# Top-32 attention and two gated blocks on one core: direct and parked tiles alternate, a second tile's down products raw, w_out split later, three places for parked scores, other orders at the start and at the end of the first block

## The reference, cut to what is computed

```python
# q, k, v: [2, 8, 576, 64]
scores = (1 / 8) * q @ k.T                      # per head, 576 x 576
kth = 32nd largest of each row
scores = where(scores >= kth, scores, -1e9)
attn = softmax(scores) ; attn_out = attn @ v
x = attn_out as [1152 tokens, 512]
h = x @ w_in                                    # 512 x 2048
y = (max(h, 0) + alpha * min(h, 0)) @ w_out     # 2048 x 512
out = ((y @ w_a) * (y @ w_b)) @ moe2_w_out      # 512 x 1536 twice, 1536 x 512
```

## Time and profile before

| | us |
|---|---|
| median of 3 runs | 652.87 |
| profiled execution | 652.81 |
| its span | 651.0 |
| DVE busy | 425.1 (65%) |
| PE busy | 606.1 (93%) |
| ACT busy | 355.6 (55%) |
| POOL busy | 291.6 (45%) |

### The profile page before, as it was taken

One profiled execution on the slowest core, in us unless ns is written; L12 is line 12 of the kernel. 1 busy time (PEld: TensorE's weight loads), 2 busy tenths in 40 slices (PEclk: granted clock), 3 DMA queues, 4 the chain that ended last, 5 costly groups with the idle time before them and its releaser, 6 DMA issues.

```text
span 651.0 us, 10894 instructions
## 1 busy us (share of the span) xinstructions
PE 606.1 (93%) x4192; PEld 507.2 (78%) x4192; DVE 425.1 (65%) x847; ACT 355.6 (55%) x642; POOL 291.6 (45%) x285
## 2 busy tenths in 40 slices
PE   5588789998999999999898989999999999999997
PEld 4366566676777878777776867899999999999996
DVE  4999999999899999999999006554221122212111
ACT  3498987877777776776676645553222112121111
POOL 0266689899978898878868660000000000000000
PEclk9877999999999999999999999999999999999999
DMA  8899972223113424332340352730011000010001
GB/s 266 316 308 350 328 267 63 73 72 87 42 59 92 132 81 127 114 112 76 114 123 29 113 167 81 263 125 1 1 49 49 0 1 1 0 50 1 0 1 48
DMA packets 30914, 68.06 MB, mean 105 GB/s; under 512 B 2704, under 2 KB 7312, under 8 KB 30736
## 3 DMA queue, kind: packets, MB, share of 16 engines
q1 hardware_dynamic: 30864, 67.38, 31.5%
HBM read 53.22 MB, written 14.16 MB: 103 GB/s over the span
## 4 chain that ended last, share of the span: by engine, by line
PE 50%; DVE 36%; POOL 8%; issue 3%; ACT 2%; DMA 1%; SPq 0%; ACTq 0%; POOLq 0%
DVE top L699 19%; DVE work L707 17%; PE ps L961 8%; PE ps L959 8%; PE ps L960 8%; PE ps L973 4%; PE ps L974 4%; PE ps L972 4%; POOL p_sb L431 2%; POOL wout_lo L418 2%; PE ps L859 2%; PE ps L861 2%; PE ps L860 2%; PE ps L891 2%; PE ps L894 1%
## 5 line engine op out<-in xcount | busy, mean ns | idle before, releaser
L699 DVE MAX8 top<-work 128x8 f32<-128x576 f32 x216 | 152.1, 746 | 0.0
L431 POOL TENSOR_TENSOR p_sb<-s_sb,p_sb 128x576 f32<-128x576 f32 x72 | 101.9, 1428 | 20.9 <-ACT p_sb L533 20.9
L752 DVE TENSOR_TENSOR ab<-ps,a_sb 128x384 f32<-128x384 f32 x36 | 20.1, 558 | 134.3 <-PE ps L961 134.3
L707 DVE MATCH_REPLACE8 work<-top,work 128x576 f32<-128x576 f32 x144 | 105.9, 744 | 0.0
L959 PE MATMUL ps<-y_parts,wab 128*128 128x384 f32 x288 | 97.2, 338 | 0.0
L961 PE MATMUL ps<-y_parts,wab 128*128 128x384 f32 x288 | 96.6, 336 | 0.0
L960 PE MATMUL ps<-y_parts,wab 128*128 128x384 f32 x288 | 96.4, 335 | 0.0
L539 ACT ACTIVATE p_sb<-p_sb,neg_max 128x576 f32<-128x576 f32 x72 | 56.3, 782 | 50.6 <-POOL p_sb L431 50.6
L859 PE MATMUL ps<-win_hi,xT_parts 128*128 128x512 f32 x144 | 59.6, 414 | 9.4 <-POOL xT_parts L448 7.3
L533 ACT ACTIVATE p_sb<-s_sb,kth_big 128x576 f32<-128x576 f32 x72 | 55.4, 787 | 11.3 <-POOL neg_max L426 11.3
L668 ACT ACTIVATE ab_hi<-ab 128x384 fp32r<-128x384 f32 x36 | 18.9, 525 | 78.0 <-DVE ab L752 78.0
(11 more groups left out here) (88 smaller groups left out, 1352.3 us busy)
## 6 DMA issues: line engine op xcount, KB each, us to landing
v_sb<-in_v SPq DMA_DIRECT2D x36, 320.0 KB, 2.9
s_dram<-keep_sb SPq DMA_DIRECT2D x16, 576.0 KB, 4.5
s_sb<-s_dram SPq DMA_DIRECT2D x16, 576.0 KB, 3.7
k_sb<-in_kT SPq DMA_DIRECT2D x24, 288.0 KB, 3.8
win_raw<-in_w_in SPq DMA_DIRECT2D x4, 1024.0 KB, 7.3
wout_raw<-in_w_out SPq DMA_DIRECT2D x4, 1024.0 KB, 9.0
wab_raw<-in_w_a SPq DMA_DIRECT2D x8, 384.0 KB, 4.0
wab_raw<-in_w_b SPq DMA_DIRECT2D x8, 384.0 KB, 6.0
```

Of the source, the lines that this page charges most:

```text
L431: nc.gpsimd.tensor_tensor(p_sb[:, chain.par, c, :], s_sb[:, chain.slot, c, :], p_sb[:, chain.par, c, :], ALU.subtract).then_inc(masked, 1)
L699: largest = nc.vector.max(top32[:, pair.par, c, 8 * r:8 * r + 8], work[:, c, :] if r else s_sb[:, pair.slot, c, :])
L707: nc.vector.match_replace(work[:, c, :], top32[:, pair.par, c, 8 * r:8 * r + 8], work[:, c, :] if r else s_sb[:, pair.slot, c, :], -3.0e38)\
```

## The change

1. **Order of the tiles.** `KINDS = "DSDPDPDPP"`: direct whole tile, split tile, then direct and parked ones in turn. Direct pairs are now 0 to 11, 16 to 19 and 24 to 27; parked ones 12 to 15, 20 to 23 and 28 to 35.
2. **Three places** for parked scores (`SLOTS = 3`). The third reaches into alpha's place, so alpha is loaded in SP's step 5 instead of 4, behind out2, once all parked stores have landed. ACT's `evict_x_turn(0)` waits for them too. `q_sb` moves behind `x_sb`.
3. **Raw down products** for the first two tiles (`RAW = 8`).
4. **w_out split** in ACT's steps 11 to 16 (POOL's 12 to 17) instead of 7 to 12 (8 to 13).
5. **Start.** Pair 0 is whole: its q is loaded first, then the two halves of its K (one per head) as two loads; its two heads go to places in different banks; the products of head 0 come first, with a semaphore of their own, and ACT copies head 0 from there.
6. **End of the first block.** `turn_x(8)` goes ahead of `down(30)`. For the last four quarters DVE computes slope and sum straight from PSUM, two operations instead of ACT's two and its own two; `halves_of_h` is gone there. The turns of y and `turn_g(35)` go ahead of the last two down products, and the last quarter's parts of g are written to the place of xT.

```diff
+RAW = 8
...
-DIRECT = (1 + WHOLE) * PAIRS
-KEPT = N_PAIRS - DIRECT
-SLOTS = 2
+KINDS = "DSDPDPDPP"
+DIRECT_PAIRS = [PAIRS * t + p for t in range(TILES) if KINDS[t] != "P" for p in range(PAIRS)]
+PARKED = [PAIRS * t + p for t in range(TILES) if KINDS[t] == "P" for p in range(PAIRS)]
+KEPT = len(PARKED)
+SLOTS = 3
...
-W_OUT_AT = {7: [0], 8: [1], 9: [2, 3], 10: [4], 11: [5, 6], 12: [7]}
-LOADS_AT = {-1: ["in1"], 0: ["in2"], 1: ["in3"], 2: ["out0"], 3: ["out1"], 4: ["alpha", "out2"], 5: ["out3"]}
+W_OUT_AT = {11: [0], 12: [1, 2], 13: [3], 14: [4, 5], 15: [6], 16: [7]}
+LOADS_AT = {-1: ["in1"], 0: ["in2"], 1: ["in3"], 2: ["out0"], 3: ["out1"], 4: ["out2"], 5: ["alpha","out3"]}
+SPLIT = KINDS.index("S")
...
-                self.split = self.tile == 0
+                self.split = self.tile == SPLIT
...
-                self.kept = number - DIRECT if number >= DIRECT else None
+                self.kept = PARKED.index(number) if number in PARKED else None
+                self.nth = DIRECT_PAIRS.index(number) if number in DIRECT_PAIRS else None
...
+        def parts_for(seq):
+
+            return (xT_hi, xT_lo) if seq == LAST_SEQ else (g_hi, g_lo)
...
                 if what == "alpha":
+                    for slot in range(SLOTS):
+                        sp.wait_ge(kept_saved[slot], 16 * len(range(slot, KEPT, SLOTS)))
                     sp.dma_start(alpha_sb[:, :], alpha).then_inc(alpha_in, 16)
...
-            for p in range(KV):
-                load_kq(pair(p))
-                load_k1(p)
-            load_qa(WHOLE + 1)
-            for p in range(KV, PAIRS):
+            sp.dma_start(q_sb[:, 0, :], qT[0]).then_inc(q0_in, 16)
+            sp.dma_start(k_sb[0:D, 0, :], kT[0, 0, 0:D]).then_inc(k0_half_in, 16)
+            sp.dma_start(k_sb[D:P, 0, :], kT[0, 0, D:P]).then_inc(kq_in[0], 16)
+            load_kq(pair(1))
+            load_k1(0)
+            load_qa(0)
+            for p in range(1, PAIRS):
                 load_k1(p)
...
-                pool.wait_ge(down_done, c // 2 + 1)
+                pool.wait_ge(down_done, RAW - QUADS + c // 2 + 1)
...
-                if turning(i) is not None and turning(i) >= QUADS:
+                if turning(i) is not None and turning(i) >= RAW:
                     lo_of_g(turning(i))
...
+                elif tile == 0:
+                    for slot in range(SLOTS):
+                        act.wait_ge(kept_saved[slot], 16 * len(range(slot, KEPT, SLOTS)))
                 nc.scalar.activation(xT_hi, src, ACT.Copy)
...
-                halves_of_h(seq)
                 if seq == LAST_UP + 1:
                     evict_y(TILES - 2)
                 hi_of_w2(2 * (seq - LAST_UP - 1) + 1)
+                if seq == LAST_SEQ:
+                    for k in range(DC):
+                        hi_of_y(0, k, FIRST_Y[k])
                 parts_of_g(seq)
-            for k, bank in enumerate((U, 1, 2, 3)):
-                hi_of_y(0, k, bank)
...
-                dve.wait_ge(u_free, up_use(seq) + 1)
-                nc.vector.tensor_tensor(neg[:, :], neg[:, :], alpha_sb[:, q * 512:(q + 1) * 512], ALU.mult)\
-                  .then_inc(slope_done, 1)
+                dve.wait_ge(u_full, up_use(seq) + 1)
+                dve.wait_ge(gt_full, seq)
+                dve.wait_ge(sum_done, LAST_UP + 1)
+                nc.vector.scalar_tensor_tensor(neg[:, :], ps[:, U, :], 0.0, alpha_sb[:, q * 512:(q + 1) * 512],
+                                               ALU.min, ALU.mult).then_inc(slope_done, 1)
                 dve.wait_ge(slope_done, seq + 1)
-                nc.vector.tensor_tensor(pos[:, :], pos[:, :], neg[:, :], ALU.subtract).then_inc(sum_done, 1)
+                nc.vector.scalar_tensor_tensor(pos[:, :], ps[:, U, :], 0.0, neg[:, :],
+                                               ALU.max, ALU.add).then_inc(u_free, 1)
...
+                if pair.number == 0:
+                    parts = ((0, 0, CUT), (0, CUT, S), (1, S - CUT, S), (1, 0, S - CUT))
+                    pe.wait_ge(k0_half_in, 16)
+                    pe.wait_ge(q0_in, 16)
...
-            down(LAST_UP - 1)
-            turn_x(TILES - 1)
-            turn_g(LAST_UP)
-            for seq in range(LAST_UP + 1, LAST_SEQ + 1):
-                up(seq)
-                down(seq - 1)
-                turn_g(seq)
...
+            turn_x(TILES - 1)
+            down(LAST_UP - 1)
+            turn_g(LAST_UP)
+            for seq in range(LAST_UP + 1, LAST_SEQ):
+                up(seq)
+                down(seq - 1)
+                turn_g(seq)
+            up(LAST_SEQ)
+            for k in range(DC):
+                turn_y(0, k, FIRST_Y[k])
+            turn_g(LAST_SEQ)
+            down(LAST_SEQ - 1)
             down(LAST_SEQ)
```

More of the change, by code:

```diff
@@ L200, in __init__ @@
                 self.tile, self.hp = divmod(number, PAIRS)
-                self.split = self.tile == 0
+                self.split = self.tile == SPLIT
                 self.j = (self.tile + 1) % 2
-                self.batch = 0 if self.split else (self.tile - 1) // WHOLE
+                self.batch = 1 if KINDS[self.tile] == "P" else 0
                 self.par, self.bound = number % 2, number % 4
-                self.slot, self.kv, self.use = number % RING, number % KV, number // KV + 1
-                self.kept = number - DIRECT if number >= DIRECT else None
+                self.slot, self.v, self.use = number % RING, number % KV, number // KV + 1
+                self.kept = PARKED.index(number) if number in PARKED else None
+                self.nth = DIRECT_PAIRS.index(number) if number in DIRECT_PAIRS else None
+                self.kv = self.nth % KV if self.kept is None else None
+                self.loads = len([m for m in PARKED if m <= number and m % RING == self.slot])
         def pair(number):
@@ L211, in direct @@
         def direct(i):
-            return Pair(i + 3) if i + 3 < DIRECT else None
+            return Pair(i + 3) if i + 3 in DIRECT_PAIRS else None
         def score_order():
@@ L218, in score_order @@
             for i in range(FIRST_STEP, LAST_STEP):
-                order += [(i + 3, 0)] if i + 3 < DIRECT else []
-                order += [(DIRECT + n, 1 - at % 2) for at, n in enumerate(AHEAD.get(i, []))]
+                order += [(i + 3, 0)] if i + 3 in DIRECT_PAIRS else []
+                order += [(PARKED[n], 1 - at % 2) for at, n in enumerate(AHEAD.get(i, []))]
             before = {}
@@ L255, in up_use, with tiles_of @@
             return (1 + QUADS) * (seq // QUADS) + 1 + seq % QUADS
+        def parts_for(seq):
+            return (xT_hi, xT_lo) if seq == LAST_SEQ else (g_hi, g_lo)
         def row(tile):
-            return (tile - 1) * P if tile else SPLIT_AT
+            if tile == SPLIT:
+                return SPLIT_AT
+            return (KINDS[:tile].count(KINDS[tile]) + (WHOLE if KINDS[tile] == "P" else 0)) * P
+        def tiles_of(t):
+            return [tile for tile in range(TILES) if row(tile) // N2 == t]
         LAST_SEQ = TILES * QUADS - 1
+        FIRST_Y = (1, 2, 3, U)
         def w2_chunk(c):
@@ L351, in _ @@
                     load_v(pair(i + 1))
-                if i > FIRST_STEP and i + 5 < DIRECT:
-                    sp.wait_ge(scored, i + 4)
+                if i > FIRST_STEP and i + 5 in DIRECT_PAIRS:
+                    sp.wait_ge(scored, pair(i + 5).nth - 1)
                     load_kq(pair(i + 5))
@@ L376, in _ @@
             sp.wait_ge(u_full, turn_use(TILES - 1) + 1)
-            for tile in range(1, 1 + TILES2):
+            for tile in tiles_of(0):
                 sp.wait_ge(y_saved[tile], 16)
@@ L389, in _ @@
                 sp.wait_ge(y_turned, t * DC)
-                for tile in ((4, 5, 6), (7, 8, 0))[t - 1]:
+                for tile in tiles_of(t):
                     sp.wait_ge(y_saved[tile], 16)
@@ L508, in copy_scores @@
                 at = SC[0]
[L509 removed]
+                act.wait_ge(scored, pair.nth + 1)
                 if pair.number >= RING:
@@ L572, in halves_of_h @@
                     for slot in range(SLOTS):
-                        act.wait_ge(kept_saved[slot], 16 * KEPT // SLOTS)
+                        act.wait_ge(kept_saved[slot], 16 * len(range(slot, KEPT, SLOTS)))
                 nc.scalar.activation(pos[:, :], ps[:, U, :], ACT.Relu)
@@ L691, in rank @@
                             if pair.kept is None:
-                                dve.wait_ge(copied, pair.u + c + 1)
+                                dve.wait_ge(copied, 2 * pair.nth + c + 1)
                             else:
-                                dve.wait_ge(s_in[pair.slot], 16 * (pair.kept // RING + 1))
+                                dve.wait_ge(s_in[pair.slot], 16 * pair.loads)
                             if c == 0 and pair.number > 1:
@@ L739, in _ @@
             for seq in range(LAST_UP + 1, LAST_SEQ + 1):
+                slope_and_sum(seq)
                 lo_of_w2(2 * (seq - LAST_UP - 1))
-                slope_and_sum(seq)
+                if seq == LAST_SEQ:
```

(19 more changed lines are left out.)

88 lines of the change are left out of this document (54 added, 34 removed).

## The result

The changed kernel takes 650.34 us (median of 7 runs, 649.1 to 651.9), the kernel before 652.96 in its 7; the ratio taken from runs side by side is 0.9946, 95% interval 0.9931 to 0.9961 (the two medians alone give 0.9960). One execution of e2 (2206 us) and one of the kernel before beside e1 to e4 (684 us) lie far off and are left out of the ratios.

What follows compares the result with a forecast made beforehand. A ranking half paced by DVE, then a matrix half paced by PE. Start -1.0, stalls -0.5 and tail -1.1 sum to -2.6 us on a median of 652.87: 650.3 us, range 647.4 to 653.6.

Steps and rivals of the forecast that it cites:

- The start: Before the first score: pair 0 no longer waits for k1_sb, PE starts 1.6 us earlier; net 1.0 us saved.
- Alpha: Alpha's load, moved to SP's step 5, lands at 89.2 instead of 84.9, making POOL's sum and PE's turn_g(0) 3.1 us late.
- The third slot: Third place for parked scores: takes away ACT's waits for parked stores, with no DVE stall behind one; worth nothing.
- DVE's stalls: Ranking half: POOL's late bounds stall DVE 2.2 us before direct pair 19, in place of 2.67; 0.5 us saved.
- rival 1: No DVE stall, as alpha is in time or PE makes up for it; -4.8 us, 648.1 us; chance 0.25.
- PE's steps: Length of PE's steps in the ranking half: 10.50 us with direct score and raw down, 9.1 in parked tile 3.
- Scores in steps 21 to 24: PE's steps 21 to 24 get scores, 9.86 us each; costed at nothing, 0.8 us if the slack behind is gone.
- Parked pairs: Pairs 20 to 23 need 17.8 to 19.3 us of the 19.3 available: no DVE stall, by little.
- The tail: Between the ranking's end and the second block: up(32) 0.7 us sooner, the end 0.2 saved; 1.1 us saved in all.
- Rival 3: Slower: alpha lands later still, past 90.8 pair 9's copy stalls DVE too; 655.1 us with alpha at 94; chance 0.12.

Runs made afterwards that it cites:

- e2: The changed kernel with two places for parked scores instead of three: 0.9970 of the kernel before.
- e1: The changed kernel with DVE's reciprocal for a finished tile behind round 3 of the ranking instead of round 1: 0.9923 of the kernel before.
- e4: The changed kernel with the old start (K of pair 0 as one load, k1_sb waited for, both heads copied at the end): 0.9966 of the kernel before.
- e3: The changed kernel with tiles in the order D S D D D P P P P, direct and parked not alternating: 1.0015 of the kernel before.
- e5: The changed kernel with the end of the first block (PE's order, ACT's halves, DVE's operations) as before: 0.9960 of the kernel before.
- e7: The changed kernel with out3 issued ahead of alpha in step 5, three places kept: 1.0004 of the kernel before.
- e8: e1 with the last direct tile one place later (pairs 28 to 31 direct): 0.9903 of the kernel before, 647.82 us.
- e6: The changed kernel with only the first tile's down products raw and w_out split in steps 7 to 12 as before: 0.9975 of the kernel before.

## Why the prediction was right, and where it was not

The time is 650.34 and the forecast was 650.3, with -2.6 us against -2.6 by the medians (-3.5 by the ratio). That the two agree to the tenth is luck: the terms that the profiles show sum to -0.83 - 0.54 - 0.95 = -2.3, and the runs spread over 2.8 us, to which the stretch at half clock can add 1.55 in some. What is right is the size of the gain and two of its three mechanisms. The terms:

- **The start**, -1.0: measured -0.83 (7.07, then 0.72 idle), and 1.1 by e4. Right, with its mechanism: PE began at 4.10 (forecast 4.0), ACT's copies 1.48 us apart where I had 1.1. The idle goes with the landing of the second half of K: 2.8 us behind its issue in e1 and e3, and no idle; 3.2 in e5, 0.17; 3.4 in e2, e7 and e8, 0.42 to 0.45; 3.7 in the changed kernel, 0.72. With the half there in time ACT's second copy follows the first at once, so the order of the products alone costs DVE nothing. The first half took 2.8 us, 288 KB before took 2.7: the sum took 2.8 and counted nothing for the halving, rightly. By the Trainium skill ("DMA: Bandwidth & Descriptors", section "Anatomy of one DMA") a half would take about 2.3 us, an estimate from its formula; the rows have 2.8 to 3.7, and that section is on DMAs issued by GpSimd, where these are issued by SyncE.
- **Alpha**, landing 89.2 and all that follows: wrong. It landed at 84.0. The step that failed is "The third slot takes away waits of ACT for parked stores; no DVE stall stands behind one, so nothing." ACT's three waits for stores, 9.9 us together, are gone, ACT is done with the last parked copy 3.4 us sooner (it starts at 72.21 instead of 75.63), and SP, which waits for that copy, issues the last store and alpha sooner: alpha at 77.36, where I had 81.92. The store also landed in 3.2 us, where I had 5.0. I asked who waits for ACT among the engines and not who waits for it in SP's list, and took SP's times over from the kernel before. The third place is not the whole of it: in e2, with two places and the three waits, that copy starts at 73.36 and alpha, issued at 80.01 when the last store has landed, lands at 87.3; in e4, with three places and the old start, the copy starts at 73.36 as well and alpha is issued at 79.04. So the new start moves it too, and of the 5.2 us by which alpha came sooner than forecast the third place makes 3.3; the rest was not taken apart. What follows from a given landing the count had about right: in e2 turn_g(0) comes at 91.7 and pair 19 stalls 1.60.
- **DVE's stalls**, 2.2 in place of 2.67: 2.13 measured, but not that stall. With alpha in time PE's step 12 began at 142.7, where rival 1 had 141.8 and the forecast 144.9; pair 17's bounds came at 188.25 (forecast 189.7) and pair 19's copy ended at 191.5, just when DVE wanted it. So far rival 1 was right. But the forecast and rival 1 alike left out a wait of DVE on POOL that stands in both lists, the reciprocal of a finished tile behind POOL's denominator, which stands behind the bounds. In the profile of before it ends an idle stretch only once, 8.6 us for the last tile behind the ranking's end, and none within the ranking. POOL's backlog peaks in step 18, with pair 19's bounds at 209.53, and the denominator of step 19 comes at 218.3 for a reciprocal that DVE reaches at 216.4. e1 shows it. The term's size was right because two errors met: 2.2 for a stall that did not come, nothing for one that did. Of the waits in DVE's list I costed only the copies.
- **PE's steps**: 10.5 (93.86 to 104.35), 9.1 in tile 3 (124.46, 133.57, 142.71, 151.83): right to 0.1, and e3 shows what they are worth. Scores in steps 21 to 24, "costed at nothing": right in the changed kernel, where DVE has no idle there, and 0.85 us once the stall of 2.13 ahead of it is gone (e1). The price that I put on it without slack was 0.8.
- **Parked pairs** 20 to 23: no stall, as forecast.
- **The tail**, -1.1: -0.95. up(32) begins 5.24 us behind the end of up(31) instead of 5.86, 0.62 of the forecast 0.7, and the end saves 0.2, as forecast. Right.
- **Rival 3** has its mechanism confirmed and its price too low: with alpha at 88.0 (e7) the stalls come to 5.05 us, where its sum, 2.2 + (alpha - 89.2), gives 1.0, and the time is that of the kernel before.

The times also hold a term that the prediction did not count, the stretches at half clock, below. How often they fall in the executions that have no profile is not known.

## What to carry to other kernels

A buffer more, or any wait taken from an engine, moves the time at which the DMA queue's list runs; work out its issue times anew before you price a load that is moved. When an engine is behind, list every wait of the bounding engine on it, the rare small ones too (a reciprocal once in four pairs), and price the one that comes due at the peak of the backlog; one such operation of 0.2 us, put half a period later, was worth 2.1 us of the ranking here (e1, 0.23% by the ratios), nearly as much as the raw tile and the later split together (e6, 0.29%). And check a right total term by term: two wrong ones can fit it.

## What the runs showed of the hardware that was not expected

- PE's granted clock fell to 0.50 (1.2 GHz) for 3.3 to 3.4 us at a time behind short idle stretches of PE: at 162 to 165.5 in the kernel before, after 2.5 us in which PE was busy for 0.74; at 354.7 to 358.0 in the changed one, after idles of 0.42 and 1.49 us. The same 1.49 us stand before up(28) in all eleven profiles, and only in three, the changed kernel, e3 and e5, did the clock fall there. It costs 1.55 us when it falls where PE sets the end (65.12 against 63.57 in e1, 66.07 in e5 against 64.52 in the kernel before). What decides it was not tried.
- The 1 MB load of alpha took 6.2 to 8.1 us with the same list ahead of it (e8, e1), and 9.7 with another 1 MB load issued just ahead of it (e7). Ordering these two the other way moved the landing of alpha by 4 us (84.0 to 88.0), although it was issued only 1 us later.
- At the program's start a load of 144 KB took as long as one of 288 KB, 2.8 against 2.7 us. A second one of 144 KB, issued 0.6 us behind it, took 2.8 to 3.7, differing from one profile to the next with the same loads around it.
